# Local attention with sinks, merged key blocks, in front of two expert stages on one Trainium2 core

## The chip, the cores and the metric

The kernel runs on one core of one Trainium2 chip. The metric is the device time of one execution in microseconds (us). Three runs of the kernel before gave 1071.53, 1071.74 and 1072.14 us, so the median is 1071.74 us.

## The reference

Three stages follow each other. Attention has 4 batches, 8 heads, 768 tokens and a head size of 64. A query sees the 128 newest keys up to itself, and the first 4 keys (the sinks). Its output feeds a dense layer pair with `h - tanh(h)` between, and that feeds a top-1 routed layer of 8 experts.

```
scores = scale * np.matmul(q, k.transpose(0, 1, 3, 2))
is_sink = pos[None, :] < int(n_sink)                 # 4
rel = pos[:, None] - pos[None, :]
in_window = (rel >= 0) & (rel < int(window))         # 128
keep = is_sink | in_window
a = softmax(np.where(keep, scores, -1e9));  x = a @ v
h = x @ w_in;  g = h - np.tanh(h);  x = g @ w_out
e_idx = argmax(x @ w_gate + bias);  out = gate * (relu(x @ w1[e]) @ w2[e])
```

## The kernel before

**Tiles.** The 3072 tokens are cut in 8 chunks of 384 tokens (`NC`), each of three tiles of 128 (`TPC`). A *pair* is one tile of queries with one pair of heads. There are 96 pairs, numbered r, 12 to a chunk; three pairs in a row, r = 3g, 3g+1, 3g+2, share a *group* g, that is a head pair and a chunk, whose queries and keys come with one load. All products use halves: a float32 tile is scaled, then split in a float16 upper part (`_hi`) and a float16 rest (`_lo`), and three products of halves stand for one of float32.

**One pair before.** A query tile of 128 rows needs the key block before it (128 columns), the 4 sinks and its own key block (128 columns), together 260 columns (`KW`). The first tile of a sequence (`is_first`) has no block before it and needs 132. TensorE writes the scores of the two heads to two PSUM banks (`s_ps`, L569). VectorE adds a mask, copies the sum to `probs` and finds the row's maximum in one instruction a head (L580). ScalarE takes the exponential (L587), VectorE inverts the row's sum (L600, L601), ScalarE scales (L607, `normed`). TensorE turns each block of 128 columns (L639, four for a pair, two for a first one), ScalarE and VectorE split the result in `pt_hi` (L644) and `pt_lo` (L648), and TensorE weighs the values (L706). Once for three pairs the sink columns are gathered (L619), turned (L662) and split (L667, L671).

**What sets the order.** Every engine has its own queue, written out by hand, and goes through it in order; semaphores tie them. First the function `alone` runs 14 pair steps without any dense product (`ALONE`). In step r, TensorE turns the probabilities of pair r-1, makes the scores of pair r+1 and weighs the values of pair r-2. A step has two half steps i = 2r and 2r+1, and tables in `conversions` and `prepare_alone` say in which half step the queries and keys of the next groups are scaled and split, the values' largest element is looked for (L477), and the weights `w_in` and `w_out` are measured (`weight_gram`, L295) and split (L357 on ScalarE, L361 and L363 on GpSimd). Then come eight *windows*, one for each chunk's dense stage. A window has 32 slots: an even slot k holds the input product `mlp_in` of block k/2+1 (12 matmuls, L751) and, between its eighth and ninth matmul, the scores of one pair and the turning of the pair of two slots ago; an odd slot holds the output product `mlp_out` (9 matmuls, L807). The remaining 82 pairs are spread over windows 0 to 6. The weight chunks that were not split in `alone` are split in window 0. Then the expert stage runs.

**The loads.** SyncE (SP) issues the loads in the order of `startup`, and holds the queue at a wait.

## Time and profile before

| | before |
|---|---|
| median of three runs | 1071.74 us |
| profiled execution | 1070.08 us |
| its span in the trace | 1068.1 us |
| TensorE busy | 989.9 us, 93% |
| VectorE busy | 650.4 us, 61% |
| ScalarE busy | 581.4 us, 54% |
| GpSimd busy | 327.3 us, 31% |

The span is the time from the first to the last instruction that the profiler saw; around it lie 2.0 us. The first matmul of the dense stage starts at 84.2 us, which is the end of `alone`. A window ends where its accumulators are copied out (VectorE, L823): at 181.7, 269.3, 359.6, 445.4, 535.6, 621.4, 704.3 and 773.9 us. In the rows, PE is TensorE's matmuls, PEld its weight loads, DVE is VectorE, ACT ScalarE, POOL GpSimd.

### The profile page before, as it was taken

Reading aid. Unit: us, or ns where it says so; the run is one execution under the profiler, and the core shown is the slowest. Engines: PE = TensorE matmul, PEld = TensorE weight load, DVE = VectorE, ACT = ScalarE, POOL = GpSimd, SP = SyncE. Lnnn points to the kernel's source line nnn. Section 1 sums busy time; section 2 is a strip of 40 time slices with the busy share of each in tenths; the row PEclk is TensorE's granted clock in tenths of the full one; section 3 lists DMA queues with packets and bytes.
Section 4 is the critical chain, followed back from the end, with each engine's and each line's share of the span. In section 5 each row is a group of like instructions: output and inputs, shape, how many; then the busy total and the mean of one; then the engine's idle time right before and its main releaser. Section 6 shows DMA issues by size and latency. Waiting matters only on the chain.

```text
span 1068.1 us, 23850 instructions
## 1 busy us (share of the span) xinstructions
PE 989.9 (93%) x7968; PEld 605.0 (57%) x7968; DVE 650.4 (61%) x2272; ACT 581.4 (54%) x1329; POOL 327.3 (31%) x462
## 2 busy tenths in 40 slices
PE   2748999999999999999999999999899999899996
PEld 1524444555554555555455556555487777677774
DVE  6665767667768767777866775646765334633331
ACT  4766786666667765766666675536422224522221
POOL 5766675112116211213511210101032232232322
PEclk9958999999999999999999999999999999999999
DMA  8710001201100320100210010041024211111111
GB/s 315 256 36 19 18 19 66 79 19 35 48 18 19 64 79 19 49 18 19 37 48 19 19 48 1 2 159 59 1 51 174 75 49 54 40 41 49 49 47 40
DMA packets 24375, 60.30 MB, mean 56 GB/s; under 512 B 9504, under 2 KB 9760, under 8 KB 22752
## 3 DMA queue, kind: packets, MB, share of 16 engines
q1 hardware_dynamic: 15392, 45.77, 13.2%
q0 software_dynamic: 5728, 13.43, 4.0%
q8 instruction: 45, 0.74, 0.3%
q10 hardware_dynamic: 3168, 0.02, 0.1%
q14 instruction: 42, 0.34, 0.1%
HBM read 45.35 MB, written 14.12 MB: 56 GB/s over the span
## 4 chain that ended last, share of the span: by engine, by line
PE 73%; DVE 12%; ACT 6%; issue 5%; POOL 1%; DVEq 1%; DMA 1%; ACTq 0%; SPq 0%; POOLq 0%
PE h_ps L751 19%; PE acc L807 18%; PE h_ps L1907 5%; PE s_ps L1856 5%; PE pt_ps L1856 5%; PE acc L1907 5%; PE pt_ps L639 4%; PE s_ps L569 3%; PE x_out L706 3%; ACT probs L587 2%; PE s_ps L858 1%; DVE qk_top L401 1%; PE pt_ps L662 1%; DVE pt_lo L648 1%; PE x_out L1833 1%
## 5 line engine op out<-in xcount | busy, mean ns | idle before, releaser
L807 PE MATMUL acc<-w_out_all,g_hi 128*128 128x512 f16 x768 | 228.4, 379 | 0.0
L751 PE MATMUL h_ps<-xt_hi,w_in_all 128*128 128x384 f16 x960 | 196.8, 328 | 4.2 <-DVE g_raw L772 3.0
L807 PE MATMUL acc<-w_out_all,g_lo 128*128 128x512 f16 x384 | 146.0, 380 | 3.3 <-DVE g_lo L792 2.7
L751 PEld LDWEIGHTS h_ps<-xt_hi,w_in_all 128*128 128x128 f16 x960 | 91.3, 100 | 62.3 <-issue 7.4
L807 PEld LDWEIGHTS acc<-w_out_all,g_hi 128*128 128x128 f16 x768 | 75.1, 98 | 77.7
L763 ACT ACTIVATE g_raw<-h_ps,batch_scale 128x384 f32<-128x384 f32 x120 | 69.5, 579 | 89.2 <-PE h_ps L751 85.3
L792 DVE SCALAR_TENSOR_TENSOR g_lo<-g_raw,batch_scale,g_hi 128x384 f16<-128x384 f32 x128 | 84.6, 661 | 44.4 <-ACT g_hi L782 44.4
L782 ACT ACTIVATE g_hi<-g_raw,batch_scale 128x384 f16<-128x384 f32 x128 | 77.9, 608 | 55.4 <-DVE g_raw L772 54.0
L101 POOL TENSOR_TENSOR tick<-tick 1x1 f32<-1x1 f32 x83 | 15.6, 188 | 293.4 <-ACT y L1923 116.2
L580 DVE CUSTOM_DVE_ANT_0 probs<-s_ps,mask 128x260 f32<-128x260 f32 (+1 forms) x192 | 70.0, 402 | 49.7 <-issue 43.9
L751 PE MATMUL h_ps<-xt_lo,w_in_all 128*128 128x384 f16 x480 | 98.3, 328 | 0.0
L644 ACT ACTIVATE pt_hi<-pt_ps 128x512 f16<-128x512 f32 (+1 forms) x96 | 53.6, 558 | 79.4 <-PE pt_ps L639 79.1
L587 ACT ACTIVATE probs<-probs,neg_max 128x260 f32<-128x260 f32 (+1 forms) x192 | 92.0, 482 | 5.7 <-DVE neg_max L580 5.7
L607 ACT ACTIVATE normed<-probs,row_sum 128x260 f32<-128x260 f32 (+1 forms) x192 | 83.6, 483 | 21.0 <-DVE row_sum L600 12.5
L772 DVE SCALAR_TENSOR_TENSOR g_raw<-h_ps,batch_scale,g_raw 128x384 f32<-128x384 f32 x120 | 73.9, 616 | 34.4 <-ACT g_raw L763 33.1
L429 POOL TENSOR_SCALAR qk_raw<-qk_raw,qk_scale 128x384 f32<-128x384 f32 (+2 forms) x62 | 37.5, 617 | 124.5 <-DVE qk_scale L420 124.3
L648 DVE TENSOR_TENSOR pt_lo<-pt_ps,pt_hi 128x512 f16<-128x512 f32 (+1 forms) x96 | 61.6, 641 | 18.2 <-ACT pt_hi L644 17.5
L1820 ACT ACTIVATE xg<-xg,x_scale 128x512 f32<-128x512 f32 x23 | 16.6, 722 | 92.1 <-DVE x_undo L1817 92.1
L639 PE MATMUL pt_ps<-ident,normed 128*128 128x128 f32 x352 | 61.7, 297 | 5.3 <-DVE pt_hi L671 3.2
L450 POOL TENSOR_TENSOR q_lo<-qk_raw,q_hi 128x384 f16<-128x384 f32 x31 | 28.4, 915 | 120.1 <-ACT q_hi L446 120.0
L751 PEld LDWEIGHTS h_ps<-xt_lo,w_in_all 128*128 128x128 f16 x480 | 47.1, 98 | 31.5 <-issue 0.7
L807 PEld LDWEIGHTS acc<-w_out_all,g_lo 128*128 128x128 f16 x384 | 37.5, 98 | 41.1 <-issue 6.2
(315 smaller groups left out, 2098.2 us busy)
## 6 DMA issues: line engine op xcount, KB each, us to landing
qk_raw<-in_qk SPq DMA_DIRECT2D x31, 454.0 KB, 3.4
...
vs_raw<-in_v SPq DMA_DIRECT2D x24, 4.0 KB
```

What stands on the lines that cost most here:

```text
L580: eng.tensor_tensor_reduce(out=probs[:, r % RING, j, cols], in0=s_banks[j][:, cols], in1=m, scale=-SCALE, scalar=3.0e38, op0=ALU.add, op1= ...
L587: eng.activation(x, x, ACT.Exp, bias=neg_max[:, r % RING, j:j + 1], scale=-1.0, accum_out=row_sum[:, r % RING, j:j + 1]).then_inc(q["exped ...
L607: eng.activation(normed[:, 2 * t + j, cols], probs[:, r % RING, j, cols], ACT.Copy, scale=total)\
L639: mm = eng.transpose(out[:, j, b - first, :], normed[:, 2 * t + j, b * KB:b * KB + P], ident[:])
L648: eng.tensor_tensor(at(pt_lo), out, at(pt_hi), ALU.subtract).then_inc(q["pt_lo_done"], 1)
L751: mm = eng.matmul(h_of(m, f), w16[0][:, f, x * DM + k * P:x * DM + (k + 1) * P], r[:, par, k, :], start=(i == 0), stop=(i == 3 * KD - 1))
L772: eng.scalar_tensor_tensor(g, h_of(m, f), batch_scale[:, b, 0:1], g, ALU.mult, ALU.subtract).then_inc(q["g_done"], 1)
L782: eng.activation(g_hi[f % 2][:], g, ACT.Copy, scale=batch_scale[:, b, 1:2]).then_inc(q["g_hi_done"], 1)
L792: eng.scalar_tensor_tensor(g_lo[f % 2][:], g, batch_scale[:, b, 1:2], g_hi[f % 2][:], ALU.mult, ALU.subtract)\
L807: mm = eng.matmul(acc[t][:, :], l[f % 2][:, t * P:(t + 1) * P], w16[1][:, f, x * DM:(x + 1) * DM], start=(f == 0 and i == 0), stop=(f == N ...
L1856: mm = eng.matmul(hid_ps[c][:, (f - 4 * c) * P:(f - 4 * c + 1) * P], w[:, k, f * P:(f + 1) * P], x[p][:, k * P:(k + 1) * P], start=(i == 0 ...
L1907: mm = eng.matmul(y_ps[bank][:, :], l[:, f * P:(f + 1) * P], rhs, start=(f == 0 and i == 0), stop=(f == KF - 1 and i == 2))
```

## The change

For a query in row p, column c of its own key block counts when c <= p, and column c of the block before counts when c > p. So of the two blocks exactly one column of each number is alive. The kernel after copies, under the predicate `later` (c > p), the scores of the block before over those of the own block, in PSUM (`copy_predicated`). What follows works on 132 columns: 4 sinks and one merged block. After the turning, GpSimd parts the merged block again in two, with zeros where a column belongs to the other (two `affine_select`, one for a first pair), into `pt`, which now has two sets. The factor 1/8 on the scores goes into the scale of the keys.

The order of `alone` is new: the queries and keys of groups 1 to 4 are converted at other half steps, the values' maxima are spread, values are weighed from step 5 on, and the next scores stand ahead of the sinks and the split on VectorE. The rest of `w_in` is now computed on VectorE in one instruction instead of on GpSimd in two. `alone` splits 7 chunks of `w_in` and 2 of `w_out`, where it split 10 and 4. Window 0 splits 9 and 14, where it split 6 and 12. Half of the next batch's value splits move to the window after. The wait ahead of the next scores is for the exponentials (`exped`), where it was for the maxima (`shifted`).

```diff
 def score_pair(E, eng, r):
-                claim_scores(eng, (q["shifted"], 2 * r + 1))
-                need(eng, q["shifted"], 2 * r)
+                claim_scores(eng, (q["exped"], 2 * r + 2))
+                need(eng, q["exped"], 2 * r)
             if E == "dve":
-                for j in range(2):
-                    eng.tensor_tensor_reduce(out=probs[:, r % RING, j, cols], in0=s_banks[j][:, cols], in1=m, scale=-SCALE,
-                                             scalar=3.0e38, op0=ALU.add, op1=ALU.min,
-                                             accum_out=neg_max[:, r % RING, j:j + 1]).then_inc(q["shifted"], 1)
+                if is_first(r):
+                    step(eng.copy_predicated(s_both[:, :, P:KW], past.unsqueeze(1).to_broadcast([P, 2, KB]),
+                                             never[:].unsqueeze(1).to_broadcast([P, 2, KB])))
+                else:
...
+                    step(eng.copy_predicated(s_both[:, :, KB:KW], past[:, SINK:KB].unsqueeze(1).to_broadcast([P, 2, P]),
+                                             s_both[:, :, 0:P]))
+                eng.tensor_reduce(neg_max[:, r % RING, :], s_both[:, :, P:KW], AX.X, ALU.max, negate=True)\
+                   .then_inc(q["shifted"], 1)
 def transpose_probs(E, eng, r):
-                    for b in range(first, 2):
-                        mm = eng.transpose(out[:, j, b - first, :], normed[:, 2 * t + j, b * KB:b * KB + P], ident[:])
+                    mm = eng.transpose(out[:, j, :], normed[:, 2 * t + j, SINK:KB], ident[:])
+            if E == "pool":
+                eng.wait_ge(q["pt_lo_done"], m + 1)
+                need(eng, q["pv_done"], pv_count(TPC * (g - 2) + (1, 2, 2)[t]))
+                eng.affine_select(out=at[:, :, 1, :], in_=both, pattern=[[0, 4], [1, P]], compare_op=ALU.is_ge, fill=0.0,
+                                  base=0, channel_multiplier=-1).then_inc(q["parted"], 1)
+                if not is_first(r):
+                    eng.affine_select(out=at[:, :, 0, :], in_=both, pattern=[[0, 4], [-1, P]], compare_op=ALU.is_gt, fill=0.0,
+                                      base=0, channel_multiplier=1).then_inc(q["parted"], 1)
 def weigh_values(E, eng, r):
-                eng.wait_ge(q["pt_lo_done"], turned(r) + (2 if last else 1))
+                eng.wait_ge(q["parted"], parts(r))
 def weight_split(E, eng, i, f):
-            if E == "pool":
+            if E == "dve" and i == 0:
+                eng.wait_ge(q["w_hi0"], f + 1)
+                eng.scalar_tensor_tensor(lo, raw, w_scale[:, 0, 0:1], hi, ALU.mult, ALU.subtract).then_inc(q["w_lo0"], 1)
+            if E == "pool" and i == 1:
 def startup(E, eng):
                 load_qk(E, eng, 0)
+                load_qk(E, eng, 1)
                 load_v(E, eng, 0)
-                eng.wait_ge(q["conv_lo"], 1)
-                load_qk(E, eng, 1)
 def conversions(E, eng, i):
-                tops = (1, 1, 1) if g == 1 else (6 * g - 9, 6 * g - 7, 6 * g - 7)
+                early = {1: (None, 0, 1, 2), 2: (4, 5, 7, 8), 3: (8, 9, 11, 12), 4: (14, 15, 17, 18)}
 def alone(E, eng):
+            weighed = {5: (1,), 6: (2,), 7: (4, 5)}
```

The first place is an even slot of window 0 on TensorE (L751 and L772 are the input product of the dense layers, L569 and L579 the scores, L639 and L646 the turning of the probabilities, L706 and L727 the values). Before:

```order
L751 MATMUL h_ps<-xt_lo,w_in_all 128x384 x4
L569 MATMUL s_ps<-k_hi,q_lo 128x260 x2
L569 MATMUL s_ps<-k_lo,q_hi 128x260 x2
L569 MATMUL s_ps<-k_hi,q_hi 128x260 x2
L639 MATMUL pt_ps<-ident,normed 128x128 x4
L751 MATMUL h_ps<-xt_hi,w_in_all 128x384 x4
```

The same slot of the kernel after:

```order
L772 MATMUL h_ps<-xt_lo,w_in_all 128x384 x4
L579 MATMUL s_ps<-k_hi,q_lo 128x260 x2
L579 MATMUL s_ps<-k_lo,q_hi 128x260 x2
L579 MATMUL s_ps<-k_hi,q_hi 128x260 x2
L646 MATMUL pt_ps<-ident,normed 128x128 x2
L772 MATMUL h_ps<-xt_hi,w_in_all 128x384 x4
```

Two of the four turnings are gone; the scores and the dense products are the same.

The second place is VectorE after the scores of pair 1 (L580 or L594 and L596: scores; L477 or L478: the values' maxima; L401: the largest query and key of group 1; L600, L601 or L612, L613: the row sums). Before:

```order
L580 ISA probs,neg_max<-s_ps,mask 128x260
L580 ISA neg_max 128x1
L477 TENSOR_REDUCE v_top<-v_raw 128x1 x2
L401 TENSOR_REDUCE qk_top<-qk_raw 128x1 x2
L412 TENSOR_SCALAR qk_exp<-qk_top 128x1
```

From the same place on, in the kernel after:

```order
L592 COPY_PREDICATED s_ps<-later,never 128x2x4
L594 COPY_PREDICATED s_ps<-later,s_ps 128x2x128
L596 TENSOR_REDUCE neg_max<-s_ps 128x2
L478 TENSOR_REDUCE v_top<-v_raw 128x1 x3
L612 TENSOR_SCALAR row_sum<-row_sum 128x2
L613 RECIPROCAL row_sum<-row_sum 128x2
L594 COPY_PREDICATED s_ps<-later,s_ps 128x2x128
L596 TENSOR_REDUCE neg_max<-s_ps 128x2
```

The scales of group 1 no longer stand between pair 1 and pair 2; they stand ahead of pair 1.

The third place is GpSimd around the conversion of group 3 (L429 or L430: scaling of queries and keys; L450 or L451: their lower halves). Before:

```order
L429 TENSOR_SCALAR qk_raw<-qk_raw,qk_scale 128x396
L361 TENSOR_SCALAR w_in_all<-w_in_all,w_scale 128x512
L363 TENSOR_TENSOR w_in_all<-w_in_all 128x512
L450 TENSOR_TENSOR q_lo<-qk_raw,q_hi 128x384
L361 TENSOR_SCALAR w_in_all<-w_in_all,w_scale 128x512
L363 TENSOR_TENSOR w_in_all<-w_in_all 128x512
L361 TENSOR_SCALAR w_in_all<-w_in_all,w_scale 128x512
L363 TENSOR_TENSOR w_in_all<-w_in_all 128x512
L450 TENSOR_TENSOR k_lo<-qk_raw,k_hi 128x396
```

After:

```order
L430 TENSOR_SCALAR qk_raw<-qk_raw,qk_scale 128x396
L534 TENSOR_TENSOR vs_all<-vs_raw,vs_all 32x512
L661 AFFINE_SELECT pt<-merged 128x4x128
L664 AFFINE_SELECT pt<-merged 128x4x128
L451 TENSOR_TENSOR q_lo<-qk_raw,q_hi 128x384
L661 AFFINE_SELECT pt<-merged 128x4x128
L664 AFFINE_SELECT pt<-merged 128x4x128
L451 TENSOR_TENSOR k_lo<-qk_raw,k_hi 128x396
```

Between the scaling and the lower half of the keys stood three chunks of `w_in`; now the parting of two pairs and the rest of the sinks' values (L534) stand there.

## Rows read from the trace of the kernel before

**Rows 1.** Busy time by stage: start, `alone` in two parts, windows 0 to 6.
```profile
core 0: us, PE busy (x) PEld busy (x) DVE busy (x) ACT busy (x) POOL busy (x), PEclk, DMA share, GB/s
8.30:25.50 17.20, 4.92 (x34) 2.73 (x35) 12.38 (x52) 8.82 (x25) 5.60 (x8) 1.00 0.95 366
25.50:84.20 58.70, 35.44 (x318) 24.39 (x318) 37.90 (x182) 41.74 (x111) 45.04 (x52) 0.72 0.40 136
84.20:181.70 97.50, 90.53 (x596) 46.82 (x597) 67.64 (x233) 70.89 (x167) 64.88 (x74) 0.98 0.09 25
181.70:269.30 87.60, 86.18 (x595) 48.16 (x594) 62.37 (x241) 56.47 (x142) 17.32 (x22) 1.00 0.15 50
269.30:359.60 90.30, 87.76 (x603) 48.51 (x602) 67.52 (x245) 59.76 (x146) 29.22 (x34) 1.00 0.13 30
359.60:445.40 85.80, 84.83 (x583) 47.38 (x581) 59.45 (x230) 54.62 (x139) 16.01 (x20) 1.00 0.15 51
```

**Rows 2.** Chain of waits in window 2: start us, us, engine, tile, line.
```profile
345.48 0.44 PE s_ps L569 x6
345.92 0.37 PE pt_ps L639 x2
...
350.62 0.59 PE pt_ps L639 x4
```

**Rows 3.** Waits of TensorE, from 84.2 to 704 us: total, times, longest.
```profile
PE pt_ps L662 <- DVE pt_lo L648: 8.1, 9, 1.2
```

**Rows 4.** Waits of TensorE in `alone`, from 8.3 to 84.2 us.
```profile
PE s_ps L569 <- POOL k_lo L450: 12.6, 4, 5.2
```

**Rows 5.** Costliest groups, shapes apart: busy us, mean ns of one, idle before.
```profile
L580 DVE CUSTOM_DVE_ANT_0 probs<-s_ps,mask 128x260 f32<-128x260 f32 x160 | 61.9, 424 | 36.3 <-issue 30.6 <-ACT normed L607 5.4
L580 DVE CUSTOM_DVE_ANT_0 probs<-s_ps,mask 128x132 f32<-128x132 f32 x32 | 8.1, 290 | 13.4 <-issue 13.3
L648 DVE TENSOR_TENSOR pt_lo<-pt_ps,pt_hi 128x512 f16<-128x512 f32 x80 | 54.8, 685 | 18.2 <-ACT pt_hi L644 17.5
L648 DVE TENSOR_TENSOR pt_lo<-pt_ps,pt_hi 128x256 f16<-128x256 f32 x16 | 6.8, 422 | 0.0
L401 DVE TENSOR_REDUCE qk_top<-qk_raw 128x1 f32<-128x384 f32 x32 | 17.4, 543 | 1.8 <-DMA qk_raw<-in_qk 1.7
L644 ACT ACTIVATE pt_hi<-pt_ps 128x512 f16<-128x512 f32 x80 | 47.6, 595 | 67.3 <-PE pt_ps L639 67.0
L644 ACT ACTIVATE pt_hi<-pt_ps 128x256 f16<-128x256 f32 x16 | 6.0, 377 | 12.1 <-PE pt_ps L639 12.1
L361 POOL TENSOR_SCALAR w_in_all<-w_in_all,w_scale 128x512 f32<-128x512 f32 x16 | 11.0, 690 | 11.7 <-ACT w_in_all L357 11.7
L363 POOL TENSOR_TENSOR w_in_all<-w_in_all 128x512 f16<-128x512 f32 x16 | 18.8, 1175 | 1.3
```

**Rows 6.** GpSimd's selects at the start: start us, us.
```profile
2.67 0.52 POOL L212 TENSOR_SCALAR_AFFINE_SELECT mask<-mask 128x384 bf16<-128x384 bf16 x1 [0.25 <-POOL table_fill L209]
3.15 0.40 POOL L215 TENSOR_SCALAR_AFFINE_SELECT mask<-mask 128x256 bf16<-128x256 bf16 x1
```

**Rows 7.** VectorE in the timeline of `alone`: pairs 0 and 2.
```profile
7.58 0.66 DVE L453 SCALAR_TENSOR_TENSOR k_lo<-qk_raw,qk_scale,k_hi 128x396 f16<-128x396 f32 x1
13.87 0.15 DVE L412 TENSOR_SCALAR qk_exp<-qk_top 128x1 int32<-128x1 int32 x1
15.24 0.15 DVE L420 TENSOR_SCALAR qk_scale<-qk_scale 128x1 int32<-128x1 int32 x1
25.52 0.29 DVE L580 CUSTOM_DVE_ANT_0 probs<-s_ps,mask 128x132 f32<-128x132 f32 x1 [1.96 <-issue]
```

**Rows 8.** Shortest, median and longest ns of line L792, all windows.
```profile
L792 DVE SCALAR_TENSOR_TENSOR g_lo<-g_raw,batch_scale,g_hi x128: 616/618/1578, 90.4 to 770.0; 128x384 f16<-128x384 f32 x128
```

**Rows 9.** VectorE and GpSimd side by side at 160 us.
```profile
159.25 1.23 DVE L792 SCALAR_TENSOR_TENSOR g_lo<-g_raw,batch_scale,g_hi 128x384 f16<-128x384 f32 x1 [1.50 <-ACT g_hi L782]
160.02 1.48 POOL L510 TENSOR_TENSOR v_lo<-v_raw,v_hi 128x512 f16<-128x512 f32 x1
```

265 lines of the change are left out of this document (144 added, 121 removed).

## The prediction

> **What bounds the kernel now.** I read the busy times by stage first, then the chain of waits, then TensorE's waits. From 84.2 us on the kernel is bound by TensorE: windows 1 to 3 last 87.6, 90.3 and 85.8 us, and it is busy for all of them but 1.4, 2.5 and 1.0 us; window 0 leaves it idle for 7.0 of 97.5 us [rows 1]. Windows 4 to 6 repeat this. So a TensorE instruction that goes from a window shortens the kernel by its full time, and one on another engine by nothing, unless TensorE waited for it. In `alone` it is the other way: TensorE is busy for 40.4 of 75.9 us, and no engine is full. VectorE is fullest in the first 17.2 us (12.4), GpSimd in the other 58.7 (45.0) [rows 1]. There the chain goes from engine to engine, and what counts is the work of the fullest and what stands ahead of the pair's next link.
>
> **Term 1, turnings in the windows.** A pair turns two blocks instead of four; a first pair turned two already. The chain has 0.37 us for two and 0.59 for four behind the same scores [rows 2], so 0.11 us a block. All pairs now turn 2, 192 in all, where there were 352, and pairs 0 to 12 turn in `alone` (44, now 26). That leaves 142 fewer in the windows: 26 in window 0, 116 in windows 1 to 6. 116 x 0.11 = 12.8 us, and 2.9 us in window 0. Nothing comes back on TensorE: scores and value products keep their sizes. The expert stage is unchanged.
>
> **Term 2, waits in the windows.** TensorE waited 9 times, 8.1 us in all, ahead of the turned sinks for `pt_lo` [rows 3]. ScalarE's copy falls from 0.60 to 0.38 us and VectorE's from 0.69 to 0.42 [rows 5]; with the 0.22 of the turning, `pt_lo` is ready 0.7 us earlier, against a mean wait of 0.9. I take 5 of the 8.1 us, 2 in window 0 (which has three of the nine waits) and 3 in the others, because VectorE's other work around the routing may still be what is late. Half a us more comes in window 0 from its other idle time of 7.0 us [rows 1]. Bounds: 0 and 15.6, all idle time of windows 0 to 6.
>
> **The unknown prices.** `copy_predicated` from PSUM to PSUM isn't in the trace. Nearest are 0.29 us for 132 columns and 0.42 for 260 [rows 5]; upwards 0.69 us, the 512 columns, if it went through twice. I take 0.42 for its 256 columns, the row of that size. The maximum over 264 columns lies between 0.29 us (132) and 0.54 (384) [rows 5]: 0.42. With the handing over, 0.89 us for both heads against 2 x (0.42 less overlap) = 0.78 before: the same. So VectorE saves per pair only the split (0.26) and two of four row-sum instructions (2 x 0.19 by their spacing), less 0.1: 0.55 us. A first pair saves little. The select on GpSimd: 0.52 us for 384 and 0.40 for 256 columns [rows 6], so 0.97 ns a column and 0.64 us for 512; two a pair. Below, 0.5; above, 1.5, the slowest two-input instruction that GpSimd shows for 512 columns [rows 9].
>
> **Term 3, the first part of `alone`.** VectorE ends the split of group 0 at 8.2 us and reaches pair 3 at 25.5 [rows 7]. In the new order it has ahead of pair 3: two maxima of group 1 (1.1), its scales (13.87 to 15.39, 1.5) [rows 7], the scores of pairs 0 to 2 (2.7, and 0.2 for the sink copies), three row sums (1.1), six maxima of values at 0.70 (4.2), their maximum (0.2), one split (0.4): 11.4 us, so pair 3 at 19.6. Before, the same things and 4 us of waiting were in these 17.3 us: for the spread of the values' scale, for the three multiplications of values on GpSimd that stood ahead of the keys of group 1. These come later now. The new load order brings group 1 before the values. I take 5 of the 5.9 us, since the exponential must end before the next scores.
>
> **Term 4, the rest of `alone`.** GpSimd, fullest with 45.0 us, loses 12 chunks at 0.69 + 1.18 = 1.87 us (22.4) [rows 5] and gains about 20 selects (12.8) and some 2 us of values: 37. VectorE has 37.9 us, loses 8 x 0.55, gains seven rests of `w_in` at 0.75 (L792's 0.62 us for 384 columns, taken to 512 [rows 8]) and the values' scale (1.2): 40. The fullest is now VectorE with 40, and 58.7 x 40/45 = 52 us if the share stays. TensorE's 12.6 us of waiting for `k_lo` [rows 4] should mostly go, since the new tables put the keys of groups 3 and 4 three half steps ahead; but what is late next is VectorE, and its links to ScalarE are serial. I take 54, a gain of 5. Bounds for terms 3 and 4 together: 0, and 17 (11.4/0.85 + 40/0.87 = 59 us, nearly all of it VectorE's work).
>
> **Term 5, window 0.** GpSimd had 64.9 us of work: six `w_in` (11.2) and three values (5.8) go, two `w_out` (3.7) and 25 selects (16) come, 68 us in over 90. Not the bound, if the order holds: a `w_out` chunk now stands five to seven slots ahead of its product. VectorE loses 7 and gains 6.8 us. So window 0 gains 2.9 + 2 + 0.5 = 5.4 us.
>
> **Waits that the change adds.** The value products wait for `parted`. The selects stand in the slot of the turning and the products two slots, some 5 us, later; they take 1.3 us. Behind a waiting select on GpSimd stand the conversions and, in window 0, `w_out`; these have slots to spare. The next scores wait for the exponentials instead of the maxima: in a window two slots lie between, so nothing; in `alone` it makes a ring of scores (0.6), copy and maximum (0.9) and exponentials (0.9), 2.4 us against 5.4 us a step now. The weighing from step 5 on only moves TensorE work that has room.
>
> **Sum.** 12.8 + 3 + 5.4 + 5 + 5 = 31.2 us. The profiled execution took 1070.1 us (its span 1068.1 and 2.0 around it), 1.7 below the median of the runs shown: 1038.9 as profiled, 1040.6 as a median.
>
> **A rule that speaks against it.** VectorE's L792 takes 0.62 us at the median and up to 1.58 [rows 8]. Near 160 us one of 1.23 us ends at 160.48, and GpSimd's L510, which started at 160.02, takes 1.48 us [rows 9]. Both have two inputs in SBUF, so these instructions stretch each other. The Trainium skill ("SBUF — State Buffer", "SBUF: two separate sides") says that GpSimd and a VectorE instruction with two SBUF inputs lock each other out of a shared port for a whole instruction; the trace agrees, with these two rows. The change puts 16 us more of GpSimd's reading into a window. If each of the 16 `g_lo` of a window stands once behind a select, VectorE gets 16 x 0.64 = 10 us, less 6.5 saved, about 4 more. Between windows 1 and 2 VectorE has 5.1 us more and TensorE idles 1.1 more [rows 1], so it costs 0.8 us a window, 6 in all, and term 2 is lost (5.5): 1052. I give that 0.08.
>
> **The rivals.** *Only the turnings pay.* The start keeps its 76 us, since the serial links and not the work bound it: what goes at GpSimd comes back at VectorE. For it: VectorE is at 65% in the longer part of `alone` and its load rises. Against it: the 12.6 us of waiting for GpSimd. 12.8 + 3 + 2.9 = 18.7: 1053. Chance 0.18.
>
> *The start shortens to what its fullest engine asks.* At 59 us instead of 76 it gains 17, 7 beyond my sum, and window 0 loses 2 us of idle more: 1032. Chance 0.14.
>
> *GpSimd becomes the bound (slower).* Its place is `alone` and window 0. With a select of p us, `alone` has 50.6 - 22.4 + 22p on GpSimd, window 0 has 51.6 + 25p. At p = 2.1 (1.48, and one L792 of 0.62 in its way each time) these are 74 and 104 us. With 10 us at the front of `alone` in which GpSimd has nothing ready, the start takes 84 and window 0 104: 8 + 6.5 us more, term 2 is lost and comes back as waits of as much: -12.8 + 14.5 + 3 = 5 us slower, 1076. It decides from about 1.9 us a select. Against it: one input, and 0.52 us for 384 columns [rows 6]. Chance 0.04.
>
> *The change does less than it says:* turnings pay, but a new wait in each window takes it again, no change. Chance 0.02.
>
> **How the numbers follow.** The forecast, 1041, has 0.54, with 1033 to 1049 as its own range. The whole range takes in both ends of the start's gain and the lock: 1026 to 1057. This leaves out the slower case, no change, and a tail on each side. A measurement of this kernel can't tell a change below 0.2% (2.1 us) from none. Faster: 0.94; the same: 0.02; slower: 0.04.
>
> **What would show it.** Right: blocks of two turnings of 0.37 us in the chain; windows 1 to 6 shorter by 2 to 3 us each; the first dense product near 74 us; no waits on `k_lo` above 1 us; the select near 0.64 us. Wrong: a select above 1.2 us; `copy_predicated` above 0.7; TensorE waiting for `pt` in a window; VectorE above 85% in `alone`.

## The result, and the profile after

| | before | after |
|---|---|---|
| median of five runs, same chip | 1072.14 us | 1064.42 us |
| lowest and highest | 1071.53, 1074.11 us | 1061.67, 1065.34 us |
| profiled execution, its span | 1070.08, 1068.1 us | 1065.34, 1063.4 us |
| VectorE, ScalarE, GpSimd busy | 650.4, 581.4, 327.3 us | 649.2, 533.0, 413.3 us |

The ratio is 0.9913, with a 95% interval of 0.99 to 0.9927. The sign of the forecast was right, its size was not: 1041 was predicted, and 1064.4 lies outside the range (1026 to 1057).

The stages of the kernel after, cut where its own pair 3 and its own windows end (they answer to [rows 1]: start in two parts, window 0, windows 1 to 3):

```profile
core 0: us, PE busy (x) PEld busy (x) DVE busy (x) ACT busy (x) POOL busy (x), PEclk, DMA share, GB/s
8.30:19.40 11.10, 4.10 (x30) 1.85 (x31) 10.12 (x33) 5.16 (x20) 4.45 (x11) 1.00 0.97 385
19.40:88.42 69.02, 36.68 (x305) 25.48 (x304) 42.74 (x143) 36.31 (x111) 40.53 (x52) 0.67 0.39 142
88.42:186.40 97.98, 89.59 (x572) 44.52 (x573) 72.82 (x179) 65.28 (x170) 71.27 (x83) 0.95 0.08 25
186.40:272.20 85.80, 83.99 (x575) 45.87 (x573) 61.21 (x184) 51.76 (x144) 38.95 (x54) 1.00 0.15 51
272.20:359.40 87.20, 85.06 (x580) 46.07 (x579) 65.57 (x186) 51.86 (x143) 37.74 (x51) 1.00 0.13 32
359.40:443.70 84.30, 83.05 (x566) 45.44 (x565) 58.92 (x173) 50.70 (x142) 34.81 (x48) 1.00 0.15 52
```

The first part of `alone` is 6.1 us shorter (pair 3's scores reach VectorE at 19.36 us, where they did at 25.5 [rows 7]), but the second part takes 69.0 us instead of 58.7. So the first dense product stands at 88.4 us, not at 84.2, and not at the 74 that was forecast. Window 0 is as long as before. Windows 1 to 3 are shorter by 1.8, 3.1 and 1.5 us. By stages, from the profiled executions of both kernels:

| | before | after | moved | predicted |
|---|---|---|---|---|
| start, up to the first dense product | 75.9 | 80.1 | +4.2 | -10.0 |
| window 0 | 97.5 | 98.0 | +0.5 | -5.4 |
| windows 1 to 6 | 522.6 | 509.5 | -13.1 | -15.8 |
| window 7 | 69.6 | 69.6 | 0 | 0 |
| expert stage and end | 294.2 | 297.9 | +3.7 | 0 |

The sum is -4.7 us for these two executions; the medians are 7.7 apart. The last row is not the change's: its code is the same, and in the other kernels below this stage took 293.7 to 296.5 us. Why the kernel after has the longest, 297.9, nothing here shows; it is counted as spread.

The chain of waits in window 2 (start us, us, what) answers to [rows 2]:

```profile
350.59 0.44 PE s_ps L579 x6
351.03 0.37 PE pt_ps L646 x2
```

Two turnings and 0.37 us stand there instead of four and 0.59. In windows 1 to 6 TensorE's turning of the pairs takes 29.4 us in all, where it took 42.5. The costliest groups, shapes apart, answer to [rows 5, 6], and give the prices that were unknown:

```profile
L661 POOL TENSOR_SCALAR_AFFINE_SELECT pt<-merged 128x512 f16<-128x512 f16 x96 | 65.3, 680 | 91.6 <-DVE merged L655 89.8 <-PE x_out L727 1.5
L596 DVE TENSOR_REDUCE neg_max<-s_ps 128x2 f32<-128x264 f32 x96 | 41.5, 432 | 3.3
L655 DVE TENSOR_TENSOR merged<-pt_ps,merged 128x256 f16<-128x256 f32 x96 | 39.7, 413 | 4.4 <-ACT merged L651 4.2 <-issue 0.3
L651 ACT ACTIVATE merged<-pt_ps 128x256 f16<-128x256 f32 x96 | 36.6, 382 | 75.7 <-PE pt_ps L646 75.2
L594 DVE COPY_PREDICATED s_ps<-later,s_ps 128x256 f32<-128x256 int32 x80 | 34.2, 428 | 47.6 <-PE s_ps L579 46.2 <-DVE dest L948 0.4
L612 DVE TENSOR_SCALAR row_sum<-row_sum 128x2 f32<-128x2 f32 x96 | 25.3, 264 | 15.6 <-ACT probs L602 12.4
```

The predicated copy takes 0.43 us (0.42 forecast), the maximum 0.43 (0.42), the two splits 0.38 and 0.41 (0.38 and 0.42), the select 0.68 at the mean (0.64). The prices were right; the time went elsewhere. TensorE's waits in `alone`, 8.3 to 84 us (total, times, longest), answer to [rows 4]:

```profile
PE s_ps L579 <- ACT probs L602: 21.7, 10, 4.3
PE pt_ps L646 <- DVE merged L655: 5.9, 4, 2.3
PE pt_ps L680 <- DVE merged L655: 5.5, 4, 2.5
PE s_ps L579 <- POOL k_lo L451: 0.9, 1, 0.9
```

The 12.6 us of waiting for `k_lo` fell to 0.9, as forecast. In their place stand 21.7 us in which the next scores wait for the exponentials, a wait to which the prediction gave no cost. The timeline shows how one of them, of 2.05 us, comes about. It lies in the longest gap between the scores of two pairs, that between pairs 4 and 5:

```profile
27.60 0.15 DVE L339 TENSOR_SCALAR v_scale<-all_exp 128x1 int32<-128x1 int32 x1
27.85 2.02 POOL L493 TENSOR_SCALAR v_raw<-v_raw,v_scale 128x512 f32<-128x512 f32 x3 [1.53 <-DVE v_scale L339]
28.58 1.96 ACT L508 ACTIVATE v_hi<-v_raw 128x512 f16<-128x512 f32 x3 [1.94 <-POOL v_raw L493]
30.79 0.36 ACT L602 ACTIVATE probs<-s_ps,neg_max 128x132 f32<-128x132 f32 x1
31.27 0.62 DVE L612 TENSOR_SCALAR row_sum<-row_sum 128x2 f32<-128x2 f32 x1 [3.52 <-ACT probs L602]
31.39 0.29 PE L579 MATMUL s_ps<-k_hi,q_lo 64*128 64x260 f16 x2 [2.05 <-ACT probs L602]
```

Pair 4's exponentials stand on ScalarE's queue behind the upper halves of the values (L508), which wait for GpSimd's scaling (L493), which waits for VectorE's scale (L339). Before, the scores had been copied out by then, and TensorE could go on. Now the pair's bank stays taken until ScalarE has got through: pair 4's scores start at 22.07 us, pair 5's at 31.39. The two longest waits of this kind have the same form. Ahead of pair 6 (3.75 us) ScalarE waits 3.04 us for GpSimd to scale the sinks' values (L517). Ahead of pair 13 (4.33 us) it waits 2.83 us for the scaling of a value block (L493), and then splits two weight chunks.

### The profile page after: what moved, and what is told of

Read it like the earlier page. It is cut to its first block, busy times and chain, and to the rows that moved or that the text cites. A ratio compares the mean times of both kernels' runs of the same rounds, so it can differ in the third digit from the quotient of the medians.

```text
span 1063.4 us, 23350 instructions
## 1 busy us (share of the span) xinstructions
PE 979.7 (92%) x7808; PEld 591.2 (56%) x7808; DVE 649.2 (61%) x1824; ACT 533.0 (50%) x1329; POOL 413.3 (39%) x605
## 4 chain that ended last, share of the span: by engine, by line
PE 70%; DVE 14%; issue 5%; ACT 4%; POOL 3%; DMA 2%; DVEq 1%; ACTq 0%; POOLq 0%; SPq 0%
PE h_ps L772 18%; PE acc L828 18%; PE pt_ps L1897 5%; PE h_ps L1948 5%; PE acc L1948 5%; PE s_ps L1897 5%; PE s_ps L579 3%; PE x_out L727 3%; PE pt_ps L646 2%; PE s_ps L879 2%; DVE g_raw L793 1%; ACT probs L602 1%; ACT g_hi L803 1%; PE s_ps L772 1%; DVE qk_top L402 1%
## 5 line engine op out<-in xcount | busy, mean ns | idle before, releaser
L772 PE MATMUL h_ps<-xt_hi,w_in_all 128*128 128x384 f16 x960 | 197.5, 329 | 5.4 <-DVE g_raw L793 3.5
L772 PEld LDWEIGHTS h_ps<-xt_hi,w_in_all 128*128 128x128 f16 x960 | 91.0, 100 | 65.2 <-issue 8.6
L784 ACT ACTIVATE g_raw<-h_ps,batch_scale 128x384 f32<-128x384 f32 x120 | 69.6, 580 | 101.8 <-PE h_ps L772 101.8
L828 PEld LDWEIGHTS acc<-w_out_all,g_hi 128*128 128x128 f16 x768 | 75.2, 98 | 77.7
L813 DVE SCALAR_TENSOR_TENSOR g_lo<-g_raw,batch_scale,g_hi 128x384 f16<-128x384 f32 x128 | 88.4, 690 | 41.9 <-ACT g_hi L803 40.5
L661 POOL TENSOR_SCALAR_AFFINE_SELECT pt<-merged 128x512 f16<-128x512 f16 x96 | 65.3, 680 | 91.6 <-DVE merged L655 89.8
L772 PE MATMUL h_ps<-xt_lo,w_in_all 128*128 128x384 f16 x480 | 99.0, 329 | 0.0
L793 DVE SCALAR_TENSOR_TENSOR g_raw<-h_ps,batch_scale,g_raw 128x384 f32<-128x384 f32 x120 | 74.0, 617 | 38.4 <-ACT g_raw L784 35.7
L619 ACT ACTIVATE normed<-probs,row_sum 128x132 f32<-128x132 f32 x192 | 66.8, 395 | 31.0 <-DVE row_sum L613 22.2
L651 ACT ACTIVATE merged<-pt_ps 128x256 f16<-128x256 f32 x96 | 36.6, 382 | 75.7 <-PE pt_ps L646 75.2
L602 ACT ACTIVATE probs<-s_ps,neg_max 128x132 f32<-128x132 f32 x192 | 68.6, 365 | 6.4 <-DVE neg_max L596 6.2
L430 POOL TENSOR_SCALAR qk_raw<-qk_raw,qk_scale 128x384 f32<-128x384 f32 (+2 forms) x62 | 37.6, 618 | 75.1 <-DVE qk_scale L421 75.1
L772 PEld LDWEIGHTS h_ps<-xt_lo,w_in_all 128*128 128x128 f16 x480 | 47.4, 99 | 31.9 <-issue 1.4
L594 DVE COPY_PREDICATED s_ps<-later,s_ps 128x256 f32<-128x256 int32 x80 | 34.2, 428 | 47.6 <-PE s_ps L579 46.2
L451 POOL TENSOR_TENSOR q_lo<-qk_raw,q_hi 128x384 f16<-128x384 f32 x31 | 29.0, 934 | 83.5 <-ACT q_hi L447 83.4
L579 PE MATMUL s_ps<-k_hi,q_lo 64*128 64x260 f16 (+1 forms) x192 | 27.5, 282 | 31.0 <-ACT probs L602 21.7
```

Of the source, the lines that this page charges most:

```text
L579: mm = eng.matmul(s_banks[j][:, cols], l[s][rows, t * P:(t + 1) * P], k[s][rows, t * KB + cols.start:t * KB + KW], start=(i == 0), stop=(i ...
L602: eng.activation(probs[:, r % RING, j, :], s_banks[j][:, P:KW], ACT.Exp, bias=neg_max[:, r % RING, j:j + 1], scale=1.0, accum_out=row_sum[ ...
L619: eng.activation(normed[:, 2 * t + j, :], probs[:, r % RING, j, :], ACT.Copy, scale=row_sum[:, r % RING, j, 0:1])\
L661: eng.affine_select(out=at[:, :, 1, :], in_=both, pattern=[[0, 4], [1, P]], compare_op=ALU.is_ge, fill=0.0, base=0, channel_multiplier=-1) ...
L772: mm = eng.matmul(h_of(m, f), w16[0][:, f, x * DM + k * P:x * DM + (k + 1) * P], r[:, par, k, :], start=(i == 0), stop=(i == 3 * KD - 1))
L784: eng.activation(g_raw[:, f % 2, :], h_of(m, f), ACT.Tanh, scale=batch_scale[:, b, 0:1]).then_inc(q["tanh_done"], 1)
```

## The experiments

Each kernel is compared with the kernel before on the same chip, whose medians were 1073.72 us (both halves, two sets of banks, values later), 1073.26 us (after both, scores first, small selects, and values later with TensorE kept busy), 1072.42 us (GpSimd kept busy, both with small selects, `w_in` rests on GpSimd) and 1072.58 us (the two rankings). The stages are from each one's profiled execution, a single one, whose total lies up to 3 us from the median. "After" is the change itself.

| kernel | median | ratio (95%) | start | window 0 | windows 1 to 6 |
|---|---|---|---|---|---|
| before | 1072.14 | | 75.9 | 97.5 | 522.6 |
| after | 1064.42 | 0.9913 (0.9900 to 0.9927) | 80.1 | 98.0 | 509.5 |
| new order alone | 1066.26 | 0.9938 (0.9916 to 0.9959) | 74.2 | 97.4 | 520.0 |
| merging alone | 1066.22 | 0.9936 (0.9913 to 0.9959) | 83.9 | 98.1 | 510.4 |
| after, two sets of banks | 1059.18 | 0.9878 (0.9854 to 0.9901) | 77.4 | 98.0 | 509.5 |
| after, values later | 1058.34 | 0.9866 (0.9840 to 0.9891) | 78.2 | 96.4 | 509.4 |
| after, both | 1056.22 | 0.9849 (0.9825 to 0.9873) | 75.3 | 95.8 | 509.5 |
| both, scores first | 1058.98 | 0.9872 (0.9856 to 0.9889) | 76.8 | 96.4 | 509.5 |
| after, small selects | 1051.07 | 0.9800 (0.9770 to 0.9829) | 78.4 | 94.0 | 504.3 |
| small selects, GpSimd kept busy | 1054.50 | 0.9828 (0.9812 to 0.9843) | 79.8 | 96.9 | 504.4 |
| both, small selects | 1046.05 | 0.9757 (0.9743 to 0.9771) | 72.2 | 93.7 | 504.3 |
| values later, TensorE kept busy | 1058.78 | 0.9861 (0.9845 to 0.9878) | 80.8 | 94.5 | 509.5 |
| both, `w_in` rests on GpSimd | 1058.80 | 0.9879 (0.9858 to 0.9899) | 76.9 | 98.5 | 509.5 |
| both, ranking from slot 24 | 1056.06 | 0.9845 (0.9832 to 0.9859) | 75.2 | 95.8 | 506.9 |
| both, ranking from slot 23 | 1052.33 | 0.9809 (0.9792 to 0.9825) | 75.2 | 96.4 | 504.4 |

**The change in its two halves.** The kernel before with the new tables and loads, but unmerged blocks and `w_in`'s rests on GpSimd. The turned probabilities have two sets here too, as in the kernel after. Of its edit:

```diff
-    pt_hi, pt_lo = (sb(n, [P, 12 + TPC, P], F16) for n in ("pt_hi", "pt_lo"))
+    pt_hi, pt_lo = ([sb(f"{n}{i}", [P, 12 + TPC, P], F16) for i in range(2)] for n in ("pt_hi", "pt_lo"))
...
-                tops = (1, 1, 1) if g == 1 else (6 * g - 9, 6 * g - 7, 6 * g - 7)
...
+                early = {1: (None, 0, 1, 2), 2: (4, 5, 7, 8), 3: (8, 9, 11, 12), 4: (14, 15, 17, 18)}
...
+            weighed = {5: (1,), 6: (2,), 7: (4, 5)}
```

> The kernel before with the new order of loads, conversions, value and weight splits and value products alone; blocks not merged, all rests on GpSimd, two sets of transposed probabilities. If the order itself is what costs (rival ORDER), its start is as late as in the kernel after (86 to 90 us). Theory RING expects the order to be good where the next scores wait only for VectorE: first dense product at 75 to 82 us, and time 1062 to 1070. Window 0 may be slow, since 14 pieces of w_out and 9 of w_in are on GpSimd there.

And the kernel after with the old tables and loads, and with `w_in`'s rests on GpSimd:

```diff
-                early = {1: (None, 0, 1, 2), 2: (4, 5, 7, 8), 3: (8, 9, 11, 12), 4: (14, 15, 17, 18)}
...
+                tops = (1, 1, 1) if g == 1 else (6 * g - 9, 6 * g - 7, 6 * g - 7)
+                splits = (2, 3) if g == 1 else (6 * g - 5, 6 * g - 3)
...
-            if E == "dve" and i == 0:
+            if E == "pool":
```

> The kernel after with the old order of the lone steps and of window 0 and the rests of w_in on GpSimd as before: the merging alone. RING: the scores wait for exponentials here too, and the old order has as many conversions ahead of them, so the start is 84 to 92 us; windows 1 to 6 shorten by 13 us as in the kernel after; window 0 grows, because GpSimd gets 16 us of selects on top of 65: 1062 to 1072. Rival ORDER: the start stays at 84 or falls, time 1052 to 1058.

The new order takes 1.7 us from the start, merging adds 8.0 (5.9 on top of the new order, there together with the rests of `w_in` on VectorE). TensorE's waits in `alone` with the new order alone, and with merging alone:

```profile
PE pt_ps L639 <- DVE pt_lo L648: 12.8, 6, 3.7
PE s_ps L569 <- POOL k_lo L450: 1.2, 1, 1.2
```

```profile
PE s_ps L576 <- POOL k_lo L448: 14.0, 4, 5.4
PE s_ps L576 <- ACT probs L599: 8.9, 8, 2.2
```

The order does what was forecast of it: the waits for `k_lo` go from 12.6 to 1.2 us. But 12.8 us of waiting for VectorE's `pt_lo` come in their place, so hardly anything is gained. The new wait for the exponentials belongs to merging, in either order.

**Whose wait is it?** In `alone`, the scores of odd pairs go to the banks of `acc0` and `h_ps`, which are free there, so that pair r+1 waits for the exponentials of pair r-1, not of r:

```diff
+            pair = s_alt if r < ALONE and r % 2 else s_both
...
-                need(eng, q["exped"], 2 * r)
+                if r < ALONE:
+                    need(eng, q["exped"], 2 * r - 2)
```

> The kernel after, but in the 14 lone steps the odd pairs write their scores to two other PSUM banks (those of the first accumulator and of the hidden tile, free at that time), so the scores of pair r+1 wait for the exponentials of pair r-1 and no longer of pair r. Theory RING (the start lost because TensorE's next scores wait for exponentials that stand in ScalarE's queue behind value and weight conversions): TensorE's 39 us of waiting for the exponentials in the lone steps falls below 10, the first dense product starts at 80 us or before (88.4 now), time 1054 to 1058. Rival QUEUE (ScalarE's and VectorE's own queues block in the same places, and the scores were only the first to show it): the wait moves to another line, the first dense product stays at 86 to 89, time 1062 to 1065.

The 39 us of that text are the 21.7 us of the matmul queue and 17.2 us of the weight loads' queue, which are largely the same time counted twice. The start is 2.7 us shorter, and the time, 1059.18 us, lies between what the two theories said. Of the 21.7 us nothing is left, but TensorE now waits for what was behind it:

```profile
PE pt_ps L651 <- DVE merged L660: 16.7, 6, 4.5
PE pt_ps L685 <- DVE merged L660: 9.2, 4, 5.7
```

So the bank was a real limit, and seven eighths of its wait were in the shadow of the serial chain scores, exponentials, sums, turning, split.

**The queue in front of the exponentials.** The first three values are split one half step later, and the sinks' too, which takes them from ahead of pair 4's exponentials:

```diff
-            if i == 7:
+            if i == 8:
                 for blk in range(TPC):
                     v_split(E, eng, 0, blk)
...
-            if i == 9:
+            if i == 10:
                 sink_halves(E, eng, 0)
```

> The kernel after with the first three value splits one half step later (behind the exponentials of pair 4 on ScalarE instead of ahead of them) and the lower half of the sinks' values likewise. RING says that the gap from the scores of pair 4 to those of pair 5 (22.1 to 31.4 us, 9.3) falls to 4 to 6 us, that from pair 5 to pair 6 (6.4) to 4 to 5, and the time by 3 to 6 us to 1058 to 1061. Rival QUEUE: the conversions then hold the next pair instead, no change (1062 to 1065).

The start gives 1.9 us, window 0 another 1.6. The gap between pairs 4 and 5 falls from 9.3 to 6.7 us, and pair 6 comes 5.1 us earlier (32.70 for 37.77). Of these 5.1 us only 1.9 reach the end of `alone`, because later waits take the rest. The 1.6 us of window 0 are TensorE's granted clock, as shown below. With the two sets of banks as well:

> The two former edits together: other PSUM banks for the odd pairs of the lone steps, and the first value splits and the sinks' values a half step later. Each alone gave the lone steps 2.7 and 1.9 us. If they remove two different links the start takes 75.5 to 76.5 us and the time is 1055 to 1057. If both remove the same 3 us of a blocked ScalarE queue, it takes 77 to 78 and the time is that of either alone, 1058 to 1059.

The two add up (2.7 + 1.9 against 4.8 us), and this kernel is faster than both kernels of the case. Putting VectorE's work on the next scores ahead of the row sums loses again:

```diff
-                    normalise(E, eng, r)
                     if r + 1 < ALONE:
                         score_pair(E, eng, r + 1)
+                    normalise(E, eng, r)
```

> As the kernel with both edits, and on VectorE the scores of pair r+1 stand ahead of the row sums of pair r, which wait for the exponentials. LINKS says that VectorE's queue was the next thing blocked (TensorE waited 16.7 us there for the split): start at 71 to 74 us, time 1051 to 1055. Rival: the row sums, and with them the turning, come 0.9 us later in each step and it is no faster or slower, 76 to 80 us.

The start is 1.5 us longer than without it, as the rival said. TensorE's turning now waits for the scaled probabilities, which wait for the row sums:

```profile
PE pt_ps L652 <- ACT normed L625: 19.2, 7, 5.2
```

**What the selects cost.** Each select treats 2 columns of a block, not 128, so that most of the probabilities are left out of the result:

```diff
-                eng.affine_select(out=at[:, :, 1, :], in_=both, pattern=[[0, 4], [1, P]], ...
+                at, both = at[:, :, :, 0:2], both[:, :, 0:2]
+                eng.affine_select(out=at[:, :, 1, :], in_=both, pattern=[[0, 4], [1, 2]], ...
```

> The kernel after with both selects cut to two columns a block, with all waits kept; the tiles that they fill are set to zero once at the start, so most of the turned probabilities are left out of the result. A select then costs 0.2 instead of 0.63 us, 9.5 us less on GpSimd in the 14 lone steps and 11 less in window 0. Theory LINKS (what the merging costs in the start is the added wait in the queues of ScalarE and VectorE, not GpSimd's volume): first dense product 86 to 89 (88.4 now), window 0 97 to 98, no change beyond 2 us. Rival VOLUME (the selects' time on GpSimd delays the conversions and the values): first dense product at 82 or before, window 0 at 94 or less, time 1050 to 1056.

The ratio falls from 0.9913 to 0.9800, which is 12 us of 1072. In the profile 1.7 go in the start, 4.0 in window 0 and 5.2 in windows 1 to 6. To part GpSimd's time from its reading, the next one fills the time with writing:

```diff
+        def fill(eng):
+            need(eng, q["filler"], filled[0])
+            filled[0] += 1
+            eng.memset(filler[:], 0.0).then_inc(q["filler"], 1)
...
                     eng.affine_select(...).then_inc(q["parted"], 1)
+                    fill(eng)
```

> The kernel after with GpSimd's selects cut to 2 columns a block (most probabilities are left out, as in the run with the small selects, 1051.1 us), and behind each small select GpSimd writes zeros to a scratch tile of 128x384 (some 0.4 us), so that it is busy in the same slots as with the full selects (0.2 + 0.4 against 0.63 us), but reads nothing and writes less than it reads before. Theory LOCK: it was GpSimd's reading of SBUF beside VectorE that cost 11 us, not GpSimd's time. Then the time stays near the small selects': 1051 to 1054, VectorE's L612 near 0.18 us at the mean in windows 1 to 5, TensorE's wait for merged near 3.5 us. Rival VOLUME: GpSimd's own work (conversions, w_out) came late behind the selects. Then window 0 and the start come back: 1059 to 1064, windows 1 to 5 unchanged. Rival ANY ACCESS: writing locks as reading does. Then L612 is back at 0.26 us and the windows too: 1060 to 1064.

GpSimd's filler in that kernel, and its window 0 (columns as above):

```profile
L676 POOL MEMSET filler<- 128x384 f32 x176 | 73.4, 417 | 0.0
```

```profile
88.08:185.00 96.92, 89.52 (x571) 44.66 (x572) 70.75 (x179) 64.91 (x170) 68.57 (x108) 0.95 0.08 25
```

The start gets 1.4 of its 1.7 us back and window 0 gets 3.0 of 4.0: there it was mostly GpSimd's time. Of the 3.0 us of window 0, 1.8 are TensorE's own busy time (89.5 us for 87.7), at a granted clock of 0.95 for 0.98, and 1.2 are idle time. Windows 1 to 6 stay at 504.4: there GpSimd's time as such costs nothing. That it is the reading, as the first theory says, does not follow, because the filler also lies at other moments than the select did (below). The ratios of the two kernels differ by 0.0028, 3 us, and their intervals overlap, so the division rests on the stages. VectorE's row-sum multiplication between 180 and 615 us in the kernel after, with small selects, and with the filler (busy us, mean ns):

```profile
L612 DVE TENSOR_SCALAR row_sum<-row_sum 128x2 f32<-128x2 f32 x62 | 16.1, 259 | 2.7
```

```profile
L612 DVE TENSOR_SCALAR row_sum<-row_sum 128x2 f32<-128x2 f32 x62 | 10.8, 174 | 2.6
```

```profile
L615 DVE TENSOR_SCALAR row_sum<-row_sum 128x2 f32<-128x2 f32 x62 | 12.9, 208 | 2.6
```

An instruction of two columns takes 0.26 us at the mean in the kernel with the full selects, 0.17 without them, and 0.62 in the row at 31.27 above, beside GpSimd's `v_lo` (L511). It stands in the chain from exponentials to the turning, once a pair.

The row sum is not the only instruction that becomes longer. Three small ones of the routing, one each a window, take 1.1, 1.1 and 1.1 us in all over windows 1 to 6 with the small selects, and 3.1, 3.7 and 3.7 with the full ones. With the filler they are back at 1.1. One of them, L945, stands ahead of VectorE's part of the dense stage (L793). In window 1 of the kernel after it ends as the select ends that began just before it:

```profile
250.19 0.63 POOL L661 TENSOR_SCALAR_AFFINE_SELECT pt<-merged 128x512 f16<-128x512 f16 x1 [0.45 <-DVE merged L655]
250.24 0.62 DVE L945 TENSOR_TENSOR work<-work,chosen 128x24 f32<-128x24 f32 x1
```

The same place with the filler, and a row sum of window 1 with the filler:

```profile
248.36 0.20 POOL L665 TENSOR_SCALAR_AFFINE_SELECT pt<-merged 128x8 f16<-128x8 f16 x1 [0.45 <-DVE merged L658]
248.41 0.18 DVE L956 TENSOR_TENSOR work<-work,chosen 128x24 f32<-128x24 f32 x1
248.51 0.42 POOL L676 MEMSET filler<- 128x384 f32 x1
```

```profile
258.92 0.42 POOL L676 MEMSET filler<- 128x384 f32 x1
259.03 0.33 DVE L615 TENSOR_SCALAR row_sum<-row_sum 128x2 f32<-128x2 f32 x1
```

L956 has begun before the writing does, so this run doesn't say what writing would do to it. The row sum that begins 0.11 us into the writing takes 0.33 us and ends with it. So writing makes a row sum longer too, and the third theory (any access) holds for that instruction. In both places VectorE's instruction ends with the long one of GpSimd that began just before it. Whether a GpSimd instruction that only writes would do the same to the routing's instructions stays open.

All three remedies together:

> The best version so far (1056.2 us) with the selects cut to 2 columns a block (most probabilities are left out). It says whether the costs found one by one add up. Two banks (2.7 us), values later (1.9) and small selects (1.7) give 6.3 us of start in sum: 80.1 - 6.3 = 73.8, just under the 74.2 of the new order without merging; window 0 95.8 - 3 to 4 = 92 to 93; windows 1 to 6 as with small selects alone: 1044 to 1047 in all. Rival OVERLAP (the same microseconds are counted twice): start stays at 75 or more, 1049 to 1052.

They give 7.9 us of start, more than the 6.3 of their sum, so nothing was counted twice. The start is then 2.0 us under that of the new order alone.

**The clock.** The kernel after enters window 0 with TensorE's clock low: the granted clock is 0.67 in the second part of `alone` (0.72 before), and 0.95 in window 0 (0.98 before). Here TensorE multiplies 128-column tiles that nobody uses, from half step 18 on (160 of them):

```diff
+                    if E == "pe" and i >= 18:
+                        eng.wait_ge(q["masked"], ALL_MASKED)
+                        for _ in range(16):
+                            eng.matmul(acc[0][:, 0:P], tri[:], ones[:], start=True, stop=True)
```

> The kernel with the values later, and 160 matmuls of 128 columns into a bank that is free, 16 behind each half step from step 9 on, so that TensorE is busy when window 0 starts. Theory CLOCK (window 0 takes 96.4 to 98 us in all versions because TensorE starts it at 1.2 GHz): its first 10 us run at 2.4 GHz, window 0 takes 92 to 94 us, the lone steps stay within 1 us of 78.2. Rival WORK (VectorE, ScalarE and GpSimd with 65 to 73 us of work each and the weight splits set window 0): it stays at 96 to 97, and the time 1058 to 1060.

```profile
8.30:89.12 80.82, 48.99 (x492) 37.13 (x493) 53.64 (x175) 41.66 (x131) 45.82 (x64) 0.83 0.47 176
89.12:183.60 94.48, 86.08 (x575) 43.60 (x573) 72.38 (x179) 64.85 (x170) 70.99 (x83) 1.00 0.09 26
```

Window 0 now runs wholly at the upper level (1.00, 2.4 GHz) and is 1.9 us shorter than with the values later alone; the start pays 2.6 us for it, and the time is no better (1058.78 for 1058.34). The first 10 us of window 0 in the kernel after, and with TensorE kept busy:

```profile
88.42:98.42 10.00, 8.43 (x32) 3.49 (x32) 3.16 (x8) 2.07 (x4) 3.32 (x3) 0.55 0.16 46
```

```profile
89.12:99.12 10.00, 8.44 (x58) 4.34 (x55) 5.04 (x13) 4.99 (x14) 5.49 (x7) 1.00 0.16 47
```

In the same busy time of 8.4 us TensorE does 32 matmuls at a granted clock of 0.55, and 58 at 1.00. With the values later it does 44 at 0.76, and before the change it did 45 at 0.77. Over the whole of window 0 TensorE is busy for 89.6 us in the kernel after, 88.0 with the values later and 86.1 when kept busy. So the low clock costs the kernel after 3.5 us in window 0. The kernel before, with nearly the clock of the values later, lost some 2 of them as well. TensorE's idle time there is the same to 0.1 us in all three, so the 1.6 us that the later values gave window 0 are all clock.

**The rest of `w_in`.** Back on GpSimd, in two instructions:

```diff
-            if E == "dve" and i == 0:
-                eng.scalar_tensor_tensor(lo, raw, w_scale[:, 0, 0:1], hi, ALU.mult, ALU.subtract)...
-            if E == "pool" and i == 1:
+            if E == "pool":
```

> The best version so far (scores in two sets of banks, values' split half a step later, 1056.2 us) with one more piece of the change undone: the rest of w_in is computed on GpSimd in two instructions (0.69 + 1.18 us), as before, not on VectorE in one (some 0.8). Theory SERIAL (what the start costs is VectorE's and ScalarE's links, not GpSimd's volume): 7 x 0.8 = 5.6 us go from VectorE in the start, of which perhaps a third is on the path: start 73 to 75.3, but window 0 gets 9 x 1.1 us more on GpSimd, so 0 to +2 there: 1054 to 1058. Rival GPSIMD (GpSimd is the fullest engine of the start and of window 0): it costs 7 x 1.87 = 13 us more there, a third of it on the path: 1060 to 1066.

It costs 1.6 us of start and 2.7 of window 0 in the profile, and the ratio rises from 0.9849 to 0.9879, 3.2 us, though the intervals overlap. The time is neither theory's, though nearer to the first's. This piece of the change pays, mostly in window 0, where GpSimd has 71 us of work with it on VectorE.

**TensorE's wait ahead of the sinks.** It stayed in windows 1 to 6 of the kernel after. Its waits from 180 to 700 us, and VectorE in the timeline of window 1 ahead of one:

```profile
PE pt_ps L680 <- DVE merged L655: 5.5, 6, 1.1
```

```profile
248.29 0.56 DVE L941 TENSOR_TENSOR counts<-s_ps,counts 128x8 f32<-128x8 f32 x3
248.88 0.18 DVE L942 TENSOR_TENSOR work<-s_ps,counts 128x24 f32<-128x24 f32 x1
249.10 0.69 DVE L631 COPY sinks<-normed 128x72 f32<-128x72 f32 x1
249.71 0.40 DVE L655 TENSOR_TENSOR merged<-pt_ps,merged 128x256 f16<-128x256 f32 x1
250.26 0.52 PE L680 MATMUL pt_ps<-ident,sinks 128*128 128x128 f32 x3 [1.12 <-DVE merged L655]
```

VectorE ranks the routing of the chunk before (L941, L942) ahead of the third pair's split. The copy of the sinks (L631) also takes 0.69 us here, beside GpSimd's scaling (L430). Two kernels move the ranking:

```diff
-            chooses, ranks = (20, 27) if late else (17, 22)
+            chooses, ranks = (20, 27) if late else (17, 24)
```

> The best version so far (scores in two sets of banks, values' split later: 1056.2 us) with one number changed: VectorE ranks a chunk's routing from slot 24 of the window on, not from slot 22, where the ranking stands ahead of VectorE's copy of the third pair's turned probabilities. Theory ROUTING (what TensorE waits for ahead of the sinks' turning is VectorE's ranking in the same slot, and the turning's saved 0.7 us could therefore not pay): TensorE's wait for merged in windows 1 to 6 falls from 5 to about 2 us, each of windows 1, 3 and 5 is 0.5 to 1 us shorter: 1053 to 1056. Rival LOCK ONLY (the wait is due to VectorE's instructions being longer beside GpSimd): no change of windows 1 to 6, 1056 to 1057. Rival SHIFT: the ranking hits the scores of slot 24 instead, and TensorE waits there as much.

And with 23 for 24:

> As the run before, with the ranking from slot 23 on: there it stands ahead of VectorE's rest of g (odd slot), with a TensorE product behind it that needs it two slots later. Theory ROUTING: as with 24, 1053 to 1056, since slot 22 is free as well. Rival SHIFT: the output product waits for g_lo, 0.3 to 0.6 us a window, and nothing is won: 1056 to 1058.

TensorE's waits from 179 to 690 us, first from slot 24, then from slot 23:

```profile
PE s_ps L585 <- issue: 3.2, 5, 0.8
...
PE pt_ps L686 <- DVE merged L661: 0.5, 1, 0.5
```

```profile
PE pt_ps L652 <- ACT normed L625: 1.4, 2, 0.7
PE pt_ps L686 <- DVE merged L661: 0.6, 1, 0.6
```

Both empty the wait (5.5 to 0.5 and 0.6 us). From slot 24 the scores wait instead (3.2 us), behind the ranking's reading of the bank that they share: in window 1 L950 ends at 244.78 us and the scores start at 244.89. The profile names no releaser for this wait. Windows 1 to 6 gain 2.6 us, which the medians don't show (1056.06 for 1056.22). From slot 23 no such wait follows, and they gain 5.1. The copy of the sinks, now ahead of GpSimd's scaling, takes 0.21 us in window 1. At 1052.33 us, with a ratio of 0.9809 to the kernel before where the change as made has 0.9913, this is the fastest kernel of the study that computes all of the reference.

This kernel also says which longer instruction does not cost the windows their time. Its row sums between 180 and 615 us:

```profile
L618 DVE TENSOR_SCALAR row_sum<-row_sum 128x2 f32<-128x2 f32 x62 | 16.4, 265 | 2.7
```

The row sums are as long as in the kernel after (265 for 259 ns), and yet windows 1 to 6 take 504.4 us, as with the small selects. So the longer row sums alone do not hold these windows at 509.5 us. What the kernel shares with the small selects and with the filler is that its L945 (here L953) takes 0.18 us again and that the wait ahead of the sinks is shorter. That these two are where the selects cost TensorE its time is argued, not shown. The selects' part and the ranking's part are in any case not separate: the wait ahead of the sinks is 3.5 us with small selects (3.3 with the filler), not 5.5. No kernel has both remedies, so whether anything is left to gain stays open.

## Why the prediction was wrong

The profiled execution took 1065.3 us against a forecast of 1038.9 for it: 26.4 us too few. The start makes 14.2 of that, window 0 5.9, windows 1 to 6 2.7, and the expert stage's own spread 3.7 (rounding leaves 0.1). The start's 14.2 us are 8.3 by which the new order alone stays behind the 10 of the forecast, and 5.9 that merging adds to it.

**Term 1, the turnings: held.** Blocks of two in the chain, at the price forecast. TensorE's turnings in windows 1 to 6 take 13.1 us less, where the term says 12.8.

**Term 2, the waits: failed.** The prediction took 3 us in windows 1 to 6, and named what could spoil it, "because VectorE's other work around the routing may still be what is late". It was: the copies in front of the sinks' turning became shorter, and the wait stayed (5.1 us in windows 1 to 6 before, 5.5 after), until the ranking left the slot. The selects take 5.2 us of these windows, and the ranking's place 5.1. Each is measured alone, and at least 2.0 us of the wait are common to both.

**Term 3, the first part: held.** Pair 3 at 19.4 us, against 19.6.

**Term 4, the rest of `alone`: the step that failed.** "The fullest is now VectorE with 40, and 58.7 x 40/45 = 52 us if the share stays." The share did not stay. VectorE did 42.7 us of work and GpSimd 40.5, near the 40 and 37 forecast, in 69 us instead of 54. The volume of the fullest engine does not set this stage. The run with the new order alone shows it: GpSimd's lateness goes, and VectorE's comes, for 1.7 us of gain. The rival in which the start keeps its 76 us had that right ("since the serial links and not the work bound it: what goes at GpSimd comes back at VectorE"), and at 1053 it still was 11 us too low.

**The wait said to cost nothing: the second failure.** "in `alone` it makes a ring of scores (0.6), copy and maximum (0.9) and exponentials (0.9), 2.4 us against 5.4 us a step now." The sum is right and answers the wrong question. A wait costs what stands ahead of the instruction it waits for, in that engine's queue: at pair 4 that is 1.96 us of ScalarE's own work and 1.94 us of its waiting for GpSimd. Merging adds 5.9 us to the start of the new order. Two sets of banks take back 2.7, the values' split behind the exponentials 1.9, the small selects 1.7, and all three 7.9. That is shown run by run. The banks and the selects belong to merging. The values' split was not tried without merging, so how much of its 1.9 us is merging's stays open.

**Term 5, window 0: failed.** It gained nothing instead of 5.4 us. "Not the bound, if the order holds" was said of GpSimd's 68 us (71.3 measured). Two things missed make up the 5.9 us. TensorE is busy for 89.6 us where 90.5 less the 2.9 of the turnings says 87.6: 1.9 us, to which the prediction gave no term. They are the clock at the window's beginning, 0.55 in its first 10 us where it was 0.77. And TensorE idles 8.4 us where the forecast has 7.0 less 2.5: 3.9 us. Of that idle time the wait ahead of the sinks is as before (3.2 us for 3.1), the wait for VectorE's g (L793) is 3.1 for 1.8, and 1.1 for exponentials and 0.5 for the parting are new. The clock and the selects are not separate: with small selects window 0 is 4.0 us shorter, and 1.9 of them are busy time, at 0.98 for 0.95.

**The lock.** The prediction gave it 0.08, with 6 us for windows 0 to 6 and the time 1052. The mechanism is there: VectorE's instructions become longer beside the selects, and with small selects 5.2 us go from windows 1 to 6. The place was wrong. It was to stretch `g_lo`, whose mean is 653 ns with small selects and 666 with full ones; what is stretched is the row sum's multiplication and three small instructions of the routing. Its example was also read too simply: the `g_lo` of 1.23 us starts at 159.25, while GpSimd's L450 runs from 159.13 to 160.07, so it was late before L510 started. The Trainium skill ("SBUF — State Buffer", "SBUF: two separate sides") names two kinds of VectorE instruction that take the shared port, those with two SBUF inputs, which meet only a GpSimd instruction that reads, and those in a two-port mode, which meet any. The prediction quoted the first kind alone. The routing's L945 has two inputs, and its 0.62 us beside a select agree with the first kind. The row sum has one input, and becomes longer beside a memset too, as the second kind would; that it runs in such a mode no run here shows.

**GpSimd as the bound, and no effect:** neither came. The slower rival's condition, a select from 1.9 us, is far from 0.68.
